# Loads, transposes and weight splits of the first batch put in another order; a prefetch and the loops of the later blocks moved

## The reference

```python
kv = einsum('bhsd,bhse->bhde', k, v)                 # q, k, v: [8, 8, 576, 64], f32
out = einsum('bhsd,bhde->bhse', q, kv)
out = out / sqrt(mean(out * out, -1) + 1e-6) * g_norm
x = out.transpose(0, 2, 1, 3).reshape(8, 576, 512)
theta = x @ w_theta
u = x + w_tok_r @ (x * cos(theta)) + w_tok_i @ (x * sin(theta))   # over the 576 tokens
x2 = u + maximum(u @ w_ch, 0)
h = maximum(x2.transpose(0, 2, 1) @ w_tok1, 0) @ w_tok2           # 576 -> 256 -> 576
u2 = x2 + h.transpose(0, 2, 1)
result = u2 + maximum(u2 @ w_ch1, 0) @ w_ch2                      # 512 -> 1536 -> 512
```

## Time and profile before

| | |
|---|---|
| runs before, median (lowest to highest of 3) | 1185.12 us (1184.59 to 1185.31) |
| the profiled execution, its own time | 1189.02 us |
| its span in the trace | 1187.2 us |
| busy share: PE, DVE, ACT, POOL | 98%, 72%, 40%, 28% |
| matmuls, and all bytes moved | 7790, 228.14 MB |
| chain that ended last: PE, issue, POOL, DVE, DMA | 65%, 15%, 9%, 6%, 3% |

### The profile page before, as it was taken

One profiled execution on the slowest core, in us unless ns is written; L12 is line 12 of the kernel. 1 busy time (PEld: TensorE's weight loads), 2 busy tenths in 40 slices (PEclk: granted clock), 3 DMA queues, 4 the chain that ended last, 5 costly groups with the idle time before them and its releaser, 6 DMA issues.

```text
span 1187.2 us, 20987 instructions
## 1 busy us (share of the span) xinstructions
PE 1160.4 (98%) x7790; PEld 1120.1 (94%) x7790; DVE 850.6 (72%) x1243; ACT 480.4 (40%) x758; POOL 330.0 (28%) x210
## 2 busy tenths in 40 slices
PE   6999999999999999999998999999999999999998
PEld 5899999999899999899997999999999999999998
DVE  3977879797978878677564676666666786666664
ACT  3623324151424233234442455555556543333331
POOL 4462525444452524231551222223200000000000
PEclk9999999999999999999999999999999999999999
DMA  9614525151625230319996787766858999999983
GB/s 287 189 26 102 120 72 127 48 130 21 159 40 155 44 80 0 83 41 310 355 314 210 242 308 277 268 231 252 292 227 313 389 312 299 251 256 311 291 201 54
DMA packets 327245, 228.14 MB, mean 192 GB/s; under 512 B 231312, under 2 KB 295184, under 8 KB 326160
## 3 DMA queue, kind: packets, MB, share of 16 engines
q1 hardware_dynamic: 324784, 227.03, 62.6%
q10 hardware_dynamic: 2400, 0.30, 0.2%
HBM read 136.84 MB, written 92.80 MB: 193 GB/s over the span
## 4 chain that ended last, share of the span: by engine, by line
PE 65%; issue 15%; POOL 9%; DVE 6%; DMA 3%; ACT 2%; SPq 0%; POOLq 0%; DVEq 0%; ACTq 0%
PE bank L1368 9%; PE bank L1370 9%; PE bank L1369 9%; PE bank L43 7%; PE bank L45 7%; PE bank L44 7%; PE bank L371 4%; PE bank L365 4%; PE bank L366 4%; POOL z_z L956 3%; PE bank L310 2%; POOL z_z L958 2%; DMA z_g<-g_scratch 1%; POOL tokens_x_token_major L949 1%; POOL weights_rms_inverse L941 1%
## 5 line engine op out<-in xcount | busy, mean ns | idle before, releaser
L365 PE MATMUL bank<-weights_tok,z_z 128*128 128x288 f32 x576 | 165.0, 301 | 1.0 <-ACT z_z L591 1.0
L366 PE MATMUL bank<-weights_tok,z_z 128*128 128x288 f32 x576 | 161.3, 294 | 0.0
L371 PE MATMUL bank<-weights_tok,z_z 128*128 128x288 f32 x576 | 125.7, 296 | 1.1 <-POOL z_z L958 0.6
L365 PEld LDWEIGHTS bank<-weights_tok,z_z 128*128 128x128 f32 x576 | 108.1, 188 | 3.2 <-ACT z_z L591 2.4
L366 PEld LDWEIGHTS bank<-weights_tok,z_z 128*128 128x128 f32 x576 | 108.2, 188 | 0.0
L371 PEld LDWEIGHTS bank<-weights_tok,z_z 128*128 128x128 f32 x576 | 92.5, 187 | 3.0 <-POOL z_z L961 2.1
L941 POOL TENSOR_TENSOR weights_rms_inverse<-weights_mean_squares,weights_minus_half 128x8 f32<-128x8 f32 x40 | 65.5, 1639 | 95.2 <-DVE weights_mean_squares L724 95.1
L956 POOL TENSOR_TENSOR z_z<-tokens_cos,z_z 128x512 fp32r<-128x512 f32 x24 | 32.0, 1331 | 184.2 <-ACT z_z L589 184.2
L596 ACT ACTIVATE weights_x_channel_major<-attention_u 128x288 fp32r<-128x288 f32 x64 | 28.5, 445 | 126.0 <-DVE attention_u L791 126.0
L43 PE MATMUL bank<-weights_x_channel_major,weights_ch 128*128 128x288 f32 x256 | 77.3, 302 | 0.0
L45 PE MATMUL bank<-weights_x_channel_major,weights_ch 128*128 128x288 f32 x256 | 75.4, 294 | 0.0
(11 more groups left out here) (297 smaller groups left out, 3639.2 us busy)
## 6 DMA issues: line engine op xcount, KB each, us to landing
g_scratch<-attention_staged SPq DMA_DIRECT2D x36, 960.0 KB, 4.3
weights_g<-g_scratch SPq DMA_DIRECT2D x24, 1152.0 KB, 10.3
g_scratch<-attention_staged SPq DMA_DIRECT2D x36, 384.0 KB, 4.8
x_scratch<-attention_u SPq DMA_DIRECT2D x8, 1152.0 KB, 4.5
u_scratch<-attention_u SPq DMA_DIRECT2D x8, 1152.0 KB, 7.5
weights_raw_u<-u_scratch SPq DMA_DIRECT2D x6, 1536.0 KB, 7.6
qkv_u_left<-u_scratch SPq DMA_DIRECT2D x12, 768.0 KB, 9.5
x_tokens_scratch<-z_x_turned SPq DMA_DIRECT2D x112, 72.0 KB, 2.0
```

The source lines that it names most:

```text
L365: pe.matmul(out, x, wtok[0][:, zt, hs], start=(i == 0), stop=False)
L366: pe.matmul(out, x, wtok[1][:, zt, hs], start=False, stop=False)
L371: mm = pe.matmul(tok_bank(b, g)[:, 0:HALF], z[1][:, zt, c * P:(c + 1) * P], wtok[0][:, zt, half * HALF:(half + 1) * HALF], start=False, st ...
```

## The change

The first batch gets its own order on PE, ACT, DVE and SP. PE begins with 24 transposes of the identity matrix. SP loads six of the eight heads of K and V first, then the left rows, q tile 0, the two other heads, q tile 1, the gain (now also as a column, `gain_col`), `w_theta`, the rest of q, and both token weights last. `kv` goes in three parts, the attention writes to four banks. The x transposes read the normed rows before the gain, and the gain is applied by `x_hi` and `x_lo`. Theta 0 and 1 go by parts between other steps. The six early `tok_weight` steps move behind theta 1, and the last six follow one another ahead of `wleft`. The loops of ACT and DVE in block a and of PE and DVE in block b are written out. The `raw_u` load is issued a batch later, and with it the splits of block c move. In block d one seed is made earlier in the first group.

```diff
+    ps_qt_first = [ps_acc[3], ps_qt]
+    ps_out_first = [*ps_out, ps_acc[0], ps_acc[1], ps_out[0]]
+    ps_kv_late = ps_acc[2]
+
+    def out_bank(n, j):
+        return ps_out_first[j] if isinstance(n, int) and n == 0 else ps_out[j % 2]
...
-        for part in range(2):
-            heads = slice(part * HP, (part + 1) * HP)
-            load_heads(kin, k, 0, heads, s_kv0[part])
-            load_heads(vin, v, 0, heads, s_kv0[part])
-        load_left(kin, k, 0, s_kv0[2])
-        load_left(vin, v, 0, s_kv0[2])
+        early, late = slice(0, 2 * (HP - 1)), slice(2 * (HP - 1), H)
+        load_heads(kin, k, 0, early, s_kv0[0])
+        load_heads(vin, v, 0, early, s_kv0[0])
+        load_left(kin, k, 0, s_kv0[1])
+        load_left(vin, v, 0, s_kv0[1])
+        load_query_tile(0, 0, s_q0[0])
+        load_heads(kin, k, 0, late, s_kv0[2])
+        load_heads(vin, v, 0, late, s_kv0[2])
+        load_query_tile(0, 1, s_q0[1])
         sp.dma_start(gn[:, :], g_norm.rearrange("(a d) -> a d", a=1).broadcast_to([P, D])).then_inc(s_raw[1], DMA)
-        for j in range(NT):
+        for side in range(2):
+            sp.dma_start(gain_col[side * D:(side + 1) * D, :], g_norm.rearrange("(d a) -> d a", a=1)).then_inc(s_raw[1], DMA)
+        sp.dma_start(raw_theta[:, :, :], w_theta.rearrange("(c p) n -> p c n", p=P)).then_inc(s_raw[0], DMA)
+        for j in range(2, NT):
             load_query_tile(0, j, s_q0[j])
-            if j == 1:
-                load_tok(w_tok_r, raw_tok[0], s_raw[3])
-        sp.dma_start(raw_theta[:, :, :], w_theta.rearrange("(c p) n -> p c n", p=P)).then_inc(s_raw[0], DMA)
+        load_tok(w_tok_r, raw_tok[0], s_raw[3])
         load_tok(w_tok_i, raw_tok[1], s_raw[4])
...
+        KV_PARTS = [(range(HP - 1), range(NJ)), (range(HP), [NJ]), ([HP - 1], range(NJ))]
...
-            wait(pe, a_qt, NT * n + j)
+            wait(pe, a_qt, NT * n + j if n > 0 else j - 1)
+            bank = ps_qt_first[j % 2] if n == 0 else ps_qt
...
-            pe.wait_ge(kv_placed, 4 * (n + 1))
-            wait(pe, d_xn, NT * n + max(j - 1, 0))
+            pe.wait_ge(kv_placed, 4 * (n + 1) + 2)
+            if isinstance(n, int) and n == 0:
+                wait(pe, d_xn, 1 if j == NJ else 0)
+            else:
+                pe.wait_ge(d_xn, NT * n + max(j - 1, 0))
...
+        def x_first_transpose(j):
+
+            pe.wait_ge(d_xn, NT if j == 3 else j + 1)
...
+            for c in range(NC):
+                mm = pe.transpose(ps_xt[j][:, c * P:(c + 1) * P], xn[j % 2][:, c * P:(c + 1) * P], ident[:, :])
...
+        def theta_part(j, w, x):
+                pe.wait_ge(d_wlo, 2)
+            for c in range(NC):
+                mm = pe.matmul(ps_theta[j][:, :], xcm[x][:, c * S + j * P:c * S + (j + 1) * P], wth[w][:, c, :],
+                               start=(w == 0 and x == 0 and c == 0), stop=(w == 1 and c == NC - 1))
+            if w == 1:
+                mm.then_inc(p_theta, 1)
...
+        WARM_UP = 24
...
+            if i < 2:
+                pe.wait_ge(d_xn, i + 3)
...
+        pe.wait_ge(s_ident, 2)
+        for _ in range(WARM_UP):
+            pe.transpose(ps_acc[0][:, 0:P], ident[:, :], ident[:, :])
         pe.wait_ge(s_zero, 2)
-        kv(0)
-        pe.wait_ge(s_ident, 2)
-
+        kv_part(0, 0)
+        kv_part(0, 1)
         q_transpose(0, 0)
+        kv_part(0, 2)
+        attend(0, 0)
         q_transpose(0, 1)
-        attend(0, 0)
         attend(0, 1)
-        for j in range(2, NT):
-            tok_weight(2 * j - 4)
-            tok_weight(2 * j - 3)
-            q_transpose(0, j)
-            if j < NT - 1:
-                attend(0, j)
+        q_transpose(0, 2)
         x_transpose(0, 0)
-        attend(0, NT - 1)
-        for j in range(NT):
-            if j + 1 < NT:
-                x_transpose(0, j + 1)
-            theta(0, j, by_parts=(j == 0))
-            tok_weight(NT + 1 + j)
-        tok_weight(2 * NT + 1)
+        attend(0, 2)
+        q_transpose(0, 3)
+        theta_part(0, 0, 0)
+        attend(0, 3)
+        q_transpose(0, 4)
+        x_transpose(0, 1)
+        theta_part(0, 0, 1)
+        attend(0, 4)
+        theta_part(1, 0, 0)
+        theta_part(0, 1, 0)
+        x_transpose(0, 2)
+        theta_part(1, 0, 1)
+        theta_part(1, 1, 0)
+        tok_weight(0)
+        tok_weight(1)
+        x_transpose(0, 3)
+        x_transpose(0, 4)
+        theta(0, 2)
+        tok_weight(2)
+        tok_weight(3)
+        theta(0, 3)
+        tok_weight(4)
+        tok_weight(5)
+        theta(0, 4)
+        for i in range(NT + 1, 2 * NT + 2):
+            tok_weight(i)
...
-        for j in range(2, NT):
-            tok_weight_hi(2 * j - 4)
-            tok_weight_hi(2 * j - 3)
-            q_copy(0, j)
-            if j == 3:
-                theta_weight_hi(0)
-            if j < NT - 1:
-                squares(0, j)
+        theta_weight_hi(0)
+        theta_weight_hi(1)
+        q_copy(0, 2)
+        act.wait_ge(s_raw[1], 3 * DMA)
         x_hi(0, 0)
-        squares(0, NT - 1)
-        theta_weight_hi(1)
+        q_copy(0, 3)
+        squares(0, 2)
+        q_copy(0, 4)
+        x_hi(0, 1)
+        squares(0, 3)
+        squares(0, 4)
+        x_hi(0, 2)
+        tok_weight_hi(0)
+        tok_weight_hi(1)
+        x_hi(0, 3)
+        x_hi(0, 4)
+        sines(0, 0)
+        tok_weight_hi(2)
+        tok_weight_hi(3)
+        sines(0, 1)
+        tok_weight_hi(4)
+        tok_weight_hi(5)
+        sines(0, 2)
+        turn_left(0)
+        for i in range(NT + 1, 2 * NT + 2):
+            tok_weight_hi(i)
 
         def body(b, first=False, more=True):
             if first:
-
-                for j in range(NT):
-                    if j + 1 < NT:
-                        x_hi(0, j + 1)
-                    if j == NJ:
-                        turn_left(0)
-                    tok_weight_hi(NT + 1 + j)
-                    if 1 <= j <= 3:
-                        sines(0, j - 1)
-                tok_weight_hi(2 * NT + 1)
                 act.wait_ge(a_left, 4)
                 act.activation(wtok[0][:, 2 * NJ, :], left_tok[:, :], ACT.Copy).then_inc(a_whi, 1)
                 act.wait_ge(d_wlo, 2)
                 z_hi(0, 0)
+                z_hi(0, 1)
                 sines(0, 3)
-                z_hi(0, 1)
                 q_copy(1, 0)
                 z_hi(0, 2)
...
-        loop(act, body, 1, B - 1)
+        for b in range(1, B - 1):
+            body(b)
...
+            if isinstance(n, int) and n == 0:
...
+                dve.wait_ge(p_kv_early, 1)
...
+                dve.wait_ge(p_kv, 1)
+                for side in range(2):
+                    hs = slice(side * D, (side + 1) * D)
+                    dve.tensor_copy(kvbd[1][hs, 1:2, hs], late[hs, 3:4, :]).then_inc(kv_placed, 1)
...
             wait(dve, g_x, NT * n + max(j - 1, 0))
+            if isinstance(n, int) and n == 0:
+                wait(dve, p_xt, max(j - 1, 0))
...
+            if isinstance(n, int) and n == 0:
...
+                dve.scalar_tensor_tensor(out=x_tile(1, j, rows(j)), in0=xt, scalar=gain_col[:, 0:1], in1=hi,
+                                         op0=ALU.mult, op1=ALU.subtract).then_inc(d_xlo, 1)
+                return
...
+        theta_weight_lo(0)
+        norm(0, 1)
+        dve.wait_ge(s_raw[1], 3 * DMA)
+        x_lo(0, 0)
+        mean_square(0, 2)
+        theta_weight_lo(1)
+        x_lo(0, 1)
+        mean_square(0, 3)
+        norm(0, 2)
+        mean_square(0, 4)
+        norm(0, 3)
+        x_lo(0, 2)
+        norm(0, 4)
+        fraction(0, 0)
+        magnitude(0, 0)
+        x_lo(0, 3)
+        x_lo(0, 4)
         tok_weight_lo(0)
         tok_weight_lo(1)
-        norm(0, 1)
-        mean_square(0, 2)
+        fraction(0, 1)
+        magnitude(0, 1)
+        rotate(0, 0)
         tok_weight_lo(2)
         tok_weight_lo(3)
-        norm(0, 2)
-        mean_square(0, 3)
+        fraction(0, 2)
+        magnitude(0, 2)
         tok_weight_lo(4)
-        x_lo(0, 0)
-        theta_weight_lo(0)
-        mean_square(0, 4)
-        norm(0, 3)
-        theta_weight_lo(1)
-        x_lo(0, 1)
-        norm(0, 4)
+        tok_weight_lo(5)
+        rotate(0, 1)
+        for i in range(NT + 1, 2 * NT + 2):
+            tok_weight_lo(i)
+        dve.wait_ge(g_x, NT)
+        fraction(0, 3)
+        magnitude(0, 3)
+        rotate(0, 2)
 
         def body(b, first=False, more=True):
             if first:
-
-                for j in range(NT):
-                    if 2 <= j + 1 < NT:
-                        x_lo(0, j + 1)
-                    if j >= 2:
-                        rotate(0, j - 2)
-                    if j < 3:
-                        fraction(0, j)
-                        magnitude(0, j)
-                    if j == NJ:
-                        fraction(0, 3)
-                        magnitude(0, 3)
-                    tok_weight_lo(NT + 1 + j)
-                tok_weight_lo(2 * NT + 1)
...
-        loop(dve, body, 1, B - 1)
```

(36 more changed lines are left out.)

## The result

| | before | with the change |
|---|---|---|
| median, us (lowest to highest) | 1185.31 (1184.59 to 1188.48, 5 runs) | 1194.31 (1192.68 to 1194.70, 5 runs) |
| ratio of the runs, 95% interval | | 1.0061 (1.0047 to 1.0074) |
| the profiled execution, and its span | 1189.02, 1187.2 | 1192.68, 1190.9 |
| busy us of PE, DVE, ACT, POOL | 1160.4, 850.6, 480.4, 330.0 | 1163.8, 852.0, 482.6, 327.6 |

The change made the kernel slower: the ratio stands for 7.2 us (5.6 to 8.8). The forecast was 1.4 us faster, and 1194.31 lies outside its range. The two profiled executions are only 3.7 us apart, about half of that; why is part of the answer.

What follows compares the result with a forecast made beforehand. PE's work bounds the steady part, so only PE's idle places were costed, the first batch's late part being DVE-bound: 3.2 - 0.84 - 2.6 - 1.15 = -1.4 us, from 1185.12 to 1183.7 us, range 1179.5 to 1187.5.

Steps and rivals of the forecast that it cites:

- First batch, +3.2: First batch: left weights split at 54.0 us, where it was 50.80, and the whole 3.2 us passes on.
- first reduction: First batch: the first reduction of the squares comes at 17.9 us, about where it was, 17.82.
- last norm: First batch: POOL sets the pace, so the last norm comes at 33.1 us in place of 33.63.
- two-bank chain: First batch: the last six token weights pass through two banks, PE, ACT, DVE, leaving DVE idle 1.6 us more.
- Loops written out ... -0.84: End of the first block's loop: DVE's 2.73 us of issue and PE's 0.84 us idle go.
- Second to third block, -2.6: Second to third block: losses of 4.6 us in place of 7.2, a saving of 2.6.
- The clock was costed at half of its fall, 0.8 us: Second to third block: of 1.6 us lost at the lower clock, half, 0.8 us, stays with the change.
- 7.2 us of loss: Second to third block before the change: PE's idle, lower clock, loop issue and short gaps together cost 7.2 us.
- Fourth block, -1.15: Fourth block, first group: the seed goes ahead of c22 and a split, so PE's 1.15 us wait goes.
- Rival D: Slower: batch 6's residual waits for the u2 store, landing past 642; +3.4 us in all, 1188.5; chance 0.10.
- my bound of +4.8: First batch's upper bound: +4.8 us with the lower clock level until 17.4 us and loads 0.5 us later.
- The gain that the prediction drew from this rule, 0.7 us: First batch: PE starts throttled and activity releases it, so the warm-up transposes would lower the sum by 0.7 us.

Runs made afterwards that it cites:

- e4: The kernel before with the new first batch alone; ratio 1.0042, +5.0 us.
- e7: As e4, but q tile 2 is loaded ahead of w_theta and copied by ACT ahead of its split; ratio 1.0026, +3.1 us against the kernel before.
- e1: The kernel before with the loops of ACT and DVE in the first block written out; ratio 1.0017, +2.0 us.
- e3: The kernel before with the raw_u load and the third block's splits moved as in the change, loops kept; ratio 1.0010, +1.2 us.
- e2: The kernel before with the loops of PE and DVE in the second block written out; ratio 1.0005, +0.6 us.
- e5: The kernel before with the one seed of the fourth block made earlier in the first group; ratio 0.9990, -1.2 us.
- e11: As e4 without the 24 identity transposes; ratio 1.0036, +4.3 us against the kernel before.
- e9: The kernel before with DVE's loop alone written out in the first block; one run, 1185.30 us beside 1187.90 before.

## Why the prediction was wrong

The forecast was -1.4 us and the change is +7.2. By the experiments the first batch accounts for 1.8 us of the miss, the loops of the first block for 2.8, and the stretch from the second to the third block for 4.4 (9.0 together, against 8.6). Point by point, against the prediction's own steps:

1. **First batch, +3.2: the mechanism right, the size too small; +5.0 by e4.** In the profile of after the end is where I put it, 54.17 for 54.0. Two errors cancelled on the way: the first reduction came 1.7 earlier than forecast and the last norm 0.8, while the two-bank chain left DVE idle 3.13 us where I took 1.6 more. The step that failed is the load order. I followed K, V and q tiles 0 and 1 to their landing, but not q tile 2 behind the 1 MB of w_theta, and so had no term for PE's wait there (1.88 us in after, 2.65 in e4) and the clock that may fall behind it (e4: left weights at 56.97). That this is what lifts the middle from 3.2 to 5.0 rests on two profiles and on e7's +3.1. The 3.2 us do pass on whole, as I wrote.
2. **"Loops written out ... -0.84": wrong in sign; +2.0 by e1.** I priced the instructions that go and nothing that their going moves. The idle at the loop's end went, but 0.37 us came in each batch, as DVE's addition now meets POOL's gain. Rows of before already showed the price: a DVE instruction of 1.55 us among its like of 0.46.
3. **Second to third block, -2.6: wrong; +1.2 by e3, +0.6 by e2.** The mechanism was right to half a us: the store lands at 644.4 in a program that runs 5.7 us later there, so at 638.7 for my 638; PE idles 3.33 for 3.6. The clock was costed at half of its fall, 0.8 us; it took 1.9 in after and 3.0 in e3. PE's wait in mix(5), 0.38 before and 1.18 in after, had no term. The larger error is in the frame. I took 7.2 us of loss from an execution 3.9 us above the median, and carried the saving over to the median, as if the surplus lay elsewhere. Most of it lay there: 39.99 us against a middle of 37.35, of which 1.1 is the longer wait for hidden_lo(7) and 1.44 the issue idle that most executions do not have.
4. **Fourth block, -1.15: right** (e5, -1.2, and the wait is gone).

That frame is also why the two profiles differ by 3.7 us and the medians by 9: the profile of before was a long one by its second to third block, that of after a short one (granted clock 0.999 over the span, 0.994 to 0.996 in its four other runs), and its first batch is one in which the clock did not fall. Rival D had the sign and one of the places, but its mechanism (a landing past 641) did not come; no rival had the port, and the first batch at +5 lies just above my bound of +4.8. The Trainium skill's rule on the clock ("TensorE: Matmul & The Clock Gate", Part 1: The HAM clock gate), that activity releases it, agrees with e11 against e4 for the kv matmuls; its other half, that idling puts it back, agrees with e4's rows at 19.41, with e11's at 18.73 and with e7's at 7.94 (behind 2.21 us of idle), while the 2.36 us of idle later in e7 left the clock up. The gain that the prediction drew from this rule, 0.7 us, did not come: e4 and e11 are 0.7 us apart the other way, inside their intervals.

## What to carry to other kernels

A term that is read from one execution must be compared with how long that same stretch takes in others before it is set against a median; if the profiled run is above the median, look first whether the surplus is in the stretch that you are about to save. When you change when an engine arrives, look for instructions that are sometimes three times as long as their like: they tell what collides, and a few tenths of a us decide who pays. And in a queue, put the transfer that someone waits for next ahead of the large one that is only wanted later.

## What the runs showed of the hardware

A DVE sum of two SBUF tiles of 128x288 took 0.45 us alone and 1.59 us when it began together with a POOL product of 1.28 us. Where both began within 0.01 us of one another, either could be the one to get through: DVE's took 0.46 us in e9 at 272.39 (and POOL's 1.61), but 1.59 in e1 at 403.65 and in e9 at 337.13. PE's wait about tile 2 left the clock up when it was 1.88 us (after) or 2.36 (e7), and was followed by the lower level when it was 2.65 (e4), but also when it was 1.80 (e11, the row at 18.73, 1.12 us for four transposes). Behind the 24 transposes 2.21 us of idle were followed by the lower level (e7), 1.38 us in after were not (row not shown: 64 matmuls of kv in 2.09 us). The length of the idle alone does not tell. And the same program, the kernel before, had medians from 1185.3 to 1188.9 us in six sessions, more than most of the parts tried here are worth, so only runs of one session were compared.
